# Placement of the pair preparation in a two-layer mixture-of-experts kernel: units moved to odd tiles, the M product's halves and the logits moved on every engine

## The reference

```python
p_packed = sm_attn(p, k, v)                # softmax(p k^T / 8) v: 32 rows per head
x = sm_attn(q, p_packed, p_packed)         # 4608 tokens x 512
h = x @ w_in                               # 4608 x 1024
solu = h * softmax(h)
y = layernorm(solu) * g_ln @ w_out         # 4608 x 512
e = argmax(y @ w_gate)                     # one of 8 experts
out = softmax(y @ w_gate)[e] * (relu(y @ w1[e]) @ w2[e])
```

## Time and profile before

| | |
|---|---|
| median of 3 executions | 1073.65 us (1069.79 to 1073.84) |
| the profiled execution's own time | 1069.79 us |
| its span, first to last instruction | 1068.2 us |
| TensorE busy | 1005.9 us, 94% of the span |
| VectorE, ScalarE, GpSimd busy | 513.4, 439.8, 287.7 us |
| mean granted TensorE clock | 0.968 |

### The profile page before, as it was taken

The page is one execution under the profiler, slowest core; times in us unless marked ns, Lnnn a source line. Parts: engine busy times, 40 slices in busy tenths (PEclk is TensorE's granted clock), DMA queues, the critical chain, the costliest instruction groups (busy, mean ns, idle before and its releaser), DMA issues.

```text
span 1068.2 us, 20090 instructions
## 1 busy us (share of the span) xinstructions
PE 1005.9 (94%) x5707; PEld 795.9 (75%) x5708; DVE 513.4 (48%) x1219; ACT 439.8 (41%) x767; POOL 287.7 (27%) x637
## 2 busy tenths in 40 slices
PE   7658999999999999999995999999999999999994
PEld 4437777777777777777773888888888888888883
DVE  3446666666666656776755423422252522244221
ACT  2345545555655656555641423312241511133120
POOL 1431222322222222265651222211221211122111
PEclk9668999999999999999997999999999999999998
DMA  9312222122232211511003731511161421111110
GB/s 354 85 46 69 90 80 89 41 90 80 90 99 89 89 42 38 197 46 49 30 31 119 276 117 49 197 39 39 39 206 39 146 99 40 39 39 49 39 39 29
DMA packets 64759, 92.62 MB, mean 87 GB/s; under 512 B 42944, under 2 KB 45120, under 8 KB 64704
## 3 DMA queue, kind: packets, MB, share of 16 engines
q1 hardware_dynamic: 55584, 61.96, 18.1%
q0 software_dynamic: 9120, 29.97, 8.1%
HBM read 70.37 MB, written 21.54 MB: 86 GB/s over the span
## 4 chain that ended last, share of the span: by engine, by line
PE 91%; ACT 2%; issue 2%; DVE 2%; DMA 1%; POOL 1%; SPq 0%; ACTq 0%; POOLq 0%; DVEq 0%
PE ps L1338 40%; PE ps L1424 13%; PE ps L1345 8%; PE ps L1403 7%; PE ps L1431 6%; PE ps L1412 3%; PE ps L1374 3%; PE ps L1303 2%; PE ps L1452 2%; PE ps L1260 2%; PE ps L1280 2%; PE ps L1269 1%; POOL w_in L440 1%; PE ps L1222 1%; PE ps L1216 1%
## 5 line engine op out<-in xcount | busy, mean ns | idle before, releaser
L1338 PE MATMUL ps<-W,xr 128*128 (+1 forms) x912 | 223.6, 400 | 2.4 <-DVE xr L1081 2.4
L1338 PE MATMUL ps<-W,zr 128*128 x912 | 222.2, 398 | 2.6 <-DVE zr L1154 2.6
L1338 PEld LDWEIGHTS ps<-W,xr 128*128 128x128 f32 x912 | 169.4, 189 | 41.5 <-DVE xr L1081 1.8
L1338 PEld LDWEIGHTS ps<-W,zr 128*128 128x128 f32 x912 | 168.3, 188 | 41.0 <-issue 2.8
L1424 PE MATMUL ps<-w_out,zr 128*128 128x512 f32 x576 | 148.0, 407 | 0.0
L1424 PEld LDWEIGHTS ps<-w_out,zr 128*128 128x128 f32 x576 | 102.7, 188 | 30.0 <-issue 7.1
L800 ACT ACTIVATE zr<-ps 128x1024 fp32r<-128x1024 f32 x38 | 39.0, 1025 | 196.6 <-PE ps L1345 196.6
L457 POOL TENSOR_TENSOR small<-half 128x1 f32<-128x1 f32 x77 | 21.4, 278 | 343.9 <-DVE yb L1166 195.6
L1081 DVE TENSOR_TENSOR xr<-ps,xr 128x512 fp32r<-128x512 f32 x39 | 26.9, 690 | 143.7 <-ACT xr L790 143.7
L795 ACT ACTIVATE hbuf<-ps 128x1024 f32<-128x1024 f32 x38 | 38.8, 1022 | 136.8 <-PE ps L1338 136.8
L1166 DVE TENSOR_SCALAR yb<-ps,gate 128x512 f32<-128x512 f32 x38 | 28.5, 751 | 137.9 <-PE ps L1338 137.9
(11 more groups left out here) (216 smaller groups left out, 1498.9 us busy)
## 6 DMA issues: line engine op xcount, KB each, us to landing
raw_e<-w_exp SPq DMA_DIRECT2D x48, 512.0 KB, 5.7
qb<-y_sorted POOLq DMA_DIRECT2D x40, 257.0 KB, 3.0
vb<-v_t SPq DMA_DIRECT2D x16, 640.0 KB, 5.3
kb<-k_t SPq DMA_DIRECT2D x16, 576.0 KB, 4.4
qb<-q_t SPq DMA_DIRECT2D x144, 64.0 KB, 3.0
y_sorted<-pad SPq DMA_DIRECT2D x8, 257.0 KB, 3.8
raw_out<-w_moe SPq DMA_DIRECT2D x4, 512.0 KB, 5.3
raw_in<-w_moe SPq DMA_DIRECT2D x4, 512.0 KB, 14.3
```

What stands on the lines that cost most here:

```text
L1338: mm = nc.tensor.matmul(dst, lhs[:, a, k * P:(k + 1) * P], rhs(b, cols), start=(first and n == 0), stop=(last and n == 2))
```

## The change

Units move from the even tiles 0, 2, 4, 6 of every nine to the odd tiles 1, 3, 5, 7, and their M products from the odd tiles to 2, 4, 6, 8. In tile 8 the next tile's `scores` are therefore put behind `up_hi`. The logits move from PSUM bank 2 to bank 7, and with them their waits. On TensorE, ScalarE and VectorE the order within an iteration is another. `m_hi` and `first_m_hi` signal once their two instructions are done rather than after each, or count by one rather than two, and `m_lo` and `first_m_lo` wait for both. All instructions and their sizes stay as they are.

```diff
-RK0 = 2 * P
-LT0, LG0 = 0, P
+LT0, LG0 = 2 * P, 3 * P
+RK0 = LT0
...
-            return (i + 1) * HP + m // 2 if 0 <= t < LAST and m % 2 == 0 and m < 8 else None
+            return (i + 1) * HP + m // 2 if 0 <= t < LAST and m % 2 == 1 and m < 8 else None
...
-            return unit_at(t - 1)
+            i, m = t // TPP, t % TPP
+            return (i + 1) * HP + m // 2 - 1 if 0 <= t < LAST and m % 2 == 0 and m > 0 else None
...  first_m_hi
-                                         ACT.Copy).then_inc(m_hi_done, 2)
+                                         ACT.Copy).then_inc(m_hi_done, 1)
...  m_hi
-                    nc.scalar.activation(m_rows(u, 0, s, slice(h * 512, (h + 1) * 512)),
-                                         ps[s * 64:(s + 1) * 64, m_bank(u), :], ACT.Copy).then_inc(m_hi_done, 1)
+                    mm = nc.scalar.activation(m_rows(u, 0, s, slice(h * 512, (h + 1) * 512)),
+                                              ps[s * 64:(s + 1) * 64, m_bank(u), :], ACT.Copy)
+                mm.then_inc(m_hi_done, 1)
...  ScalarE's iteration
+                if there(t):
+                    exp_h(t)
+                if there(t - 1):
+                    copy_lt(t - 1)
+                if u is not None:
+                    k_exp(u)
                 if v is not None:
                     m_hi(v, 0)
+                if there(t):
+                    squares(t)
+                if u is not None:
+                    k_et(u)
+                if there(t + 1):
+                    a_hi(t + 1)
                 if there(t - 1):
-                    copy_lt(t - 1)
-                if there(t):
-                    exp_h(t)
-                if u is not None:
-                    k_exp(u)
-                    k_et(u)
+                    exp_l(t - 1)
                 if v is not None:
                     m_hi(v, 1)
-                if there(t + 1):
-                    a_hi(t + 1)
-                if there(t):
-                    squares(t)
-                if there(t - 1):
-                    exp_l(t - 1)
...  first_m_lo
+                dve.wait_ge(m_hi_done, 2 * u + 2)
                 for s in range(2):
-                    dve.wait_ge(m_hi_done, 4 * u + 2 * s + 2)
...  m_lo
+                dve.wait_ge(m_hi_done, 2 * u + h + 1)
                 cols = slice(h * 512, (h + 1) * 512)
                 for s in range(2):
-                    dve.wait_ge(m_hi_done, 4 * u + 2 * h + s + 1)
...  VectorE's iteration
+                if there(t + 1):
+                    sum_s(t + 1)
                 if u is not None:
                     k_max(u)
-                if v is not None:
-                    m_lo(v, 0)
-                if there(t + 1):
-                    sum_s(t + 1)
-                if there(t - 1):
-                    pick(t - 1)
                 if there(t):
                     solu(t)
                     row_sum(t)
+                if v is not None:
+                    m_lo(v, 0)
+                if u is not None:
+                    k_sum(u)
+                if there(t - 1):
+                    pick(t - 1)
                 if there(t + 1):
                     a_lo(t + 1)
+                if u is not None:
+                    k_pp(u)
                 if v is not None:
                     m_lo(v, 1)
-                if u is not None:
-                    k_sum(u)
-                    k_pp(u)
...  turn_a, turn_z, logits_t
-                wait(pe, rank_read, t - 2)
+                if t >= 2:
+                    pe.wait_ge(pick_chain, 4 * (t - 2) + 1)
...
-                if t >= 1:
-                    pe.wait_ge(pick_chain, 4 * (t - 1) + 1)
...
+                wait(pe, rank_read, t)
...  TensorE's iteration
-                if there(t + 1):
+                late = v is not None and (t + 1) % TPP == 0
+                if there(t + 1) and not late:
                     scores(t + 1)
...
                     up_hi(t)
+                if late:
+                    scores(t + 1)
+                if there(t):
                     up_lo(t)
                 if u is not None:
                     k_scores(u, t)
+                if there(t - 1):
+                    down_hi(t - 1, range(0, 3))
+                    logits_t(t - 1)
+                    down_hi(t - 1, range(3, 6))
                 if v is not None:
                     m_half(v, 0)
                 if there(t - 1):
-                    logits_t(t - 1)
-                    down_hi(t - 1, range(0, 4))
                     turn_logits(t - 1)
-                    down_hi(t - 1, range(4, KF))
+                    down_hi(t - 1, range(6, KF))
+                if u is not None:
+                    k_turn(u)
+                if there(t - 1):
+                    down_lo(t - 1, range(0, 3))
+                if there(t + 1):
+                    turn_a(t + 1)
                 if v is not None:
                     m_half(v, 1)
                 if u is not None:
-                    k_turn(u)
+                    k_pack(u)
                 if there(t - 1):
-                    down_lo(t - 1, range(0, 4))
-                if there(t + 1):
-                    turn_a(t + 1)
-                if there(t - 1):
-                    down_lo(t - 1, range(4, KF))
-                if u is not None:
-                    k_pack(u)
+                    down_lo(t - 1, range(3, KF))
```

More of the change, by code:

```diff
@@ L199, in moe_kernel @@
         g_ps = ps[:, 7, :]
-        l_ps = ps[:, 2, :]
         constants_set, zeroed, small_weights_in, numbers_set, numbers_cast, blanks_set = map(
@@ L730, in copy_lt @@
                 wait(act, logits_turned, t)
-                nc.scalar.activation(lt[:], l_ps[:, LT0:LT0 + P], ACT.Copy).then_inc(logits_copied, 1)
+                nc.scalar.activation(lt[:], g_ps[:, LT0:LT0 + P], ACT.Copy).then_inc(logits_copied, 1)
             def exp_l(t):
@@ L1022, in pick @@
                 dve.wait_ge(logits_turned, t + 1)
-                nc.vector.tensor_reduce(lg[:], l_ps[:, LG0:LG0 + P].rearrange("p (k e) -> p e k", k=4)[:, 0:E, :],
+                nc.vector.tensor_reduce(lg[:], g_ps[:, LG0:LG0 + P].rearrange("p (k e) -> p e k", k=4)[:, 0:E, :],
                                         AX.X, ALU.add).then_inc(pick_chain, 1)
@@ L1451, in logits_t @@
                     g = 32 * (k % 4)
-                    mm = nc.tensor.matmul(l_ps[g:g + 32, LT0:LT0 + P], wog[:, k, :], zraw[:, k * P:(k + 1) * P],
+                    mm = nc.tensor.matmul(g_ps[g:g + 32, LT0:LT0 + P], wog[:, k, :], zraw[:, k * P:(k + 1) * P],
                                           start=(k < 4), stop=(k >= 4))
@@ L1457, in turn_logits @@
                 pe.wait_ge(logits_copied, t + 1)
-                nc.tensor.transpose(l_ps[:, LG0:LG0 + P], lt[:], ident[:]).then_inc(logits_turned, 1)
+                nc.tensor.transpose(g_ps[:, LG0:LG0 + P], lt[:], ident[:]).then_inc(logits_turned, 1)
             def rank(t):
```

## The result

The changed kernel takes 1097.2 us (median of 4, 1095.89 to 1097.94) against 1072.46 for the kernel before (4 executions, 1069.79 to 1073.84): ratio 1.0232, 95% interval 1.0207 to 1.0257. It is 24.7 us slower; 1092 was forecast, in a range of 1080 to 1104. Two executions of variants further down, 1452.36 and 1450.45 us at a mean granted clock of 0.648, are left out of their medians and ratios.

A forecast was written before the change was run, and what follows sets the result against it. TensorE, busy 439.92 of 440.00 us, was taken as the bound. Terms 10.3 + 6.3 + 3.1 + 1.0 + 0.7 - 1.4 = 20.0 us gave 1089.8 from the profiled execution, 1093.7 from the median; forecast 1092, range 1080 to 1104.

The forecast's parts named there:

- ordinary M tiles: Nine M products: the second m_half waits for m_lo, costing TensorE 1.14 us each with restart, 10.3 us in all.
- last tiles: Tile 8, three times: scores behind up_hi delay exp_h, so TensorE waits from turn_logits on; 2.1 us each, 6.3 in all.
- units: Twelve units: added changes of array form and k_pack's wait for k_et cost 0.26 us each, 3.1 us in all.
- start: Before tile 0: the last first_m_lo waits for both copies and holds up max_s behind it, 1.0 us.
- tile 0: Tile 0 loses its unit and tile 1 gets one; the sum of both grows by 0.7 us, bounds 0 to 3.1.
- end: At the second stage's end the logits' wait for z_raw shrinks, z_hi being made one copy earlier: -1.4 us.
- What bounds it: Second stage: TensorE is full, so ending waits wins nothing and each wait it feels adds time; possible gain under 0.5%.
- B: M products: the waits are hidden, leaving about 3 us, 1077, the same; chance 0.08.
- C: Second stage: TensorE's clock falls after the twelve waits, 1136, or 1104 with a quarter of it; chance 0.07.
- D: Logits: their 36 form changes into and out of the narrow array are hidden, 6.5 us less, 1070 or 1067; chance 0.04.
- E: ScalarE's queue: copy_lt behind exp_h delays turn_logits up to 0.5 us in the last nine tiles, k_pack up to 1.1; 1109.

The follow-up runs named there:

- two experiments: Changed kernel, once with VectorE's pick ahead of m_lo(v, 0), 1099.46 us; once with the logits back in PSUM bank 2 and their old waits, 1092.68 us.
- the experiment that widened the room to 3.82 us: Changed kernel with the logits back in PSUM bank 2 and the second m_half behind all of down_lo: 1086.65 us, ratio 1.0133.
- the two signals: Changed kernel with m_hi and first_m_hi signalling after each copy again, m_lo and first_m_lo waiting for one at a time: 1091.77 us, ratio 1.0195.
- an experiment with longer waits: Changed kernel with VectorE's pick ahead of m_lo of the first half in tiles with an M product: 1099.46 us, ratio 1.0256.

## Why the prediction was right

*The sum.* The range and the main mechanism held, and the sum was short: 20.0 us were added up for the profiled execution, and 27.9 were measured. The 1092 also stood 2.2 above the sum's 1089.8, between two bases. By term, forecast and measured: ordinary M tiles 10.3 and 13.8, last tiles 6.3 and 7.7, units 3.1 and 3.0, start 1.0 and 1.0, tile 0 0.7 and 2.0, end -1.4 and -0.5, expert stage 0 and 0.8.

*What bounds it.* Right. TensorE was full, and every wait of the new order is in the time.

*Ordinary M tiles.* Forecast 1.14 each, 10.3 in nine; measured 1.53 (14.27 of tile 24 against 12.74), 13.8. The mechanism was right and its last link was missed. The waiter is not the second half of M: `turn_a`'s new wait reads `4 * (t - 2) + 1`, but it is called for t+1, so it means this iteration's `pick`, which the forecast does not mention. The link costs 0.4, as two experiments show from two sides. The rest is confirmed twice: with the link taken out the tile is 1.12 longer than before, where 1.14 was forecast, and the experiment that widened the room to 3.82 us saw the chain of 3.57 (3.64 forecast) fit into it.

*The pair's last tile.* Forecast 2.1, measured 2.56: tiles 16 and 17 take 30.09 for 27.28, less 0.25 for the unit. The wait for `copy_lt` is 0.87, where 1.0 was worked out, and `z_raw` at 4.22 us was forecast at 4.1. The missed link is here too: the wait is 1.19 for `pick`, and without the link the tile is 0.40 shorter.

*Units.* Forecast 0.26, measured 0.24 to 0.25, but by two errors that cancel, which is luck. One narrow block more between wide matmuls costs 0.19, leaving and entering, and only 0.09 was counted; the place of `k_pack` and its wait cost 0.05, and 0.17 was counted. The Trainium skill ("TensorEngine Tiling (Array Packing)", Key Properties) says that a changed tiling mode drains the engine. The rows agree that a change costs time. The Trainium skill ("TensorE: Matmul & The Clock Gate", Single matmul latency) puts the drain at some 175 ns. The 0.19 measured is for two changes, so it is near one such drain, not two.

*Start.* 1.0 forecast, 1.0 measured (0.97), and undone by the two signals.

*Tile 0.* Forecast 0.7; measured 2.0: the first pair is longer by 10.1 where the others are longer by 8.2. Tile 0 fell to 11.66, between the bounds, but tile 1 then took 15.60 for a steady unit tile's 14.78. Its clock is 0.54 in its first 2 us and 1.00 from 94.1 us on, since tile 0 with its 3.1 us of idle time has a low one (0.65 in its window). The forecast priced the chain and not the clock. Each figure is of one execution: in the profiles of variants that leave tile 0 alone it takes 10.15 us at a clock of 0.84 or 12.42 at 0.64, and before it takes 13.78 at 0.78 or 12.66 at 0.85. Tile 1 is 15.6 or more in all that have it.

*End.* Forecast -1.4, measured -0.5. From the last `up_hi` to the last rank the kernel won 1.25 (18.13 for 19.38 us), and then lost 1.0 before the first expert product, where the sorted rows' DMA landed later. That loss is seen, not explained. Nor does the gain have the forecast's cause alone (`z_hi` made one copy earlier than `z_raw`): TensorE's wait behind the last tile did fall from 2.00 for `z_raw` to 1.08 for `z_hi`, but in the two variants of the kernel before that moved the logits without the rest of the order it is 2.1. The rest of the new order is needed for it; in both variants TensorE waits 0.54 to 0.55 for `solu` there, in the changed kernel not at all. A likely reason, not tested, is that `exp_h` stands ahead of `copy_lt` only in the changed kernel.

*Rivals.* B fell with the twelve waits. C did not happen in this kernel, and an experiment with longer waits showed it can. D fell: the logits' new place costs 0.19 in a unit tile and hides nothing in the others (12.74 and 11.37 as before). E's 0.5 us in the last nine tiles did not come (plain tiles of 11.35, no wait of `turn_logits`); why not, no run tells.

## What to carry over

Where one engine is full, an edit of the order is worth the difference of two lengths: the chain from the product that fills a shared buffer to its last reader, and what the full engine can do meanwhile. Write down both, with every wait's counter resolved to the iteration in which it is called, and with what stands in front of the reader on its own queue. Signalling once for two instructions looks like a saving of one wait and here costs 0.6 us of a chain in which TensorE stands, nine times.

## What the hardware showed

The expert stage, with the same instructions, takes mostly one of two lengths in the twelve profiles. The windows of it in the kernel before and in the run with the logits in bank 2:

```profile
573.58:1068.20 494.62, 477.94 (x2280) 389.83 (x2280) 154.19 (x214) 134.34 (x154) 100.09 (x231) 0.99 0.25 83
```
```profile
595.68:1094.20 498.52, 481.83 (x2280) 392.67 (x2280) 154.13 (x214) 134.40 (x154) 100.56 (x231) 0.98 0.25 83
```

In four of the ten other profiles it is the long one too, 498.1 to 498.3 us, with a short stretch of half clock in its second tile (14.07 us at 0.88 for 12.53 at 1.00) and another near its end; one profile has only the latter, 497.3; the other five take 494.6 to 495.4. No part of these kernels differs there. So 3 to 4 us come from where the clock happens to fall. That is as much as the executions of the kernel before are apart (1069.79 to 1073.84), though one profile to a kernel can't show that it is the same thing. A gain of 2 us in another stage is read from its tiles, not from the total.
